# Attention inputs turned by VectorE instead of TensorE, head pair by head pair, in a fused attention and mixer kernel

## The chip, the cores and the metric

One core of one Trainium2 chip runs the whole program. The metric is the device time of one execution in microseconds. The kernel is timed as a median of several runs, and one execution is profiled.

## What is computed

Three layers, one after the other, for 4 batches of 768 positions. First a linear attention with a decay for every channel (8 heads of 48 channels), then an MLP mixer (over positions, then over channels), then a channel mix with a shift by one position.

```python
def _attn_ref(q, k, v, alpha):            # each (4, 8, 768, 48)
    for t in range(S):
        state = alpha[:, :, t, :, None] * state + np.einsum('bhd,bhe->bhde', k[:, :, t], v[:, :, t])
        y[:, :, t] = np.einsum('bhd,bhde->bhe', q[:, :, t], state)

def _moe_ref(x, w_tok1, w_tok2, w_ch1, w_ch2):    # x (4, 768, 384)
    u = x + (np.maximum(x.transpose(0, 2, 1) @ w_tok1, 0.0) @ w_tok2).transpose(0, 2, 1)
    return u + np.maximum(u @ w_ch1, 0.0) @ w_ch2

def _moe2_ref(x, mu_k, mu_r, w_k, w_v, w_r):
    xk = mu_k * x + (1.0 - mu_k) * x_prev         # x_prev is x one position earlier
    xr = mu_r * x + (1.0 - mu_r) * x_prev
    k = np.maximum(xk @ w_k, 0.0)
    return 1.0 / (1.0 + np.exp(-(xr @ w_r))) * (k * k @ w_v)
```

## The kernel before

Every engine has its own program, written out by hand. Nothing is scheduled; what stands in a program runs in that order, and semaphores tie the programs together.

**Steps.** The attention of one batch is cut into 24 steps: 6 chunks of 128 positions (`NC`) by 4 head pairs (`NP`). One step works on 128 positions of two heads, 96 channels (`W2`). `step(i)` gives chunk `i // 4` and head pair `i % 4`, so the four head pairs of a chunk follow each other and a state is needed again only four steps later. A step goes through these functions:

- TensorE `transposes` (L508): three matmuls with the identity turn q, k and alpha of the step, each from 128 positions x 96 channels to 96 x 128, into one bank. It raises `tr_done`.
- VectorE `scans` (L914, L916) makes running products of alpha forwards and backwards, `scale_qk` (L923, L926, L929) multiplies q and k by them into `qkd` and raises `qkd_ready`.
- ScalarE `spread_q` (L769 twice, L773) rounds q (for each head) and k to the high halves `qs_hi` and `ks_hi`; VectorE `split_low` (L939 twice, L943) makes the low halves `qs_lo` and `ks_lo`.
- TensorE `attention_scores`: a transpose of k (L522) and three matmuls (L530). It raises `scores_done`.
- VectorE `mask` (L949) copies the scores under the causal mask into `am`; ScalarE `store_kdt` (L763) copies the turned k.
- TensorE `attention_out`: scores times v (L546), q times state (L550, not in the first chunk) and k times v (L553, not in the last). It raises `y_done`.
- ScalarE `high_x` (L759) and VectorE `outputs` (L960 or L963 for the state, L968 for the low half of the result), then GpSimd `own_head` (L420) clears the other head's part of the state.

The first batch (`r = 0`) runs alone, with two banks for each kind of tile. Its part of the code stays as it is but for the signatures of the helper functions.

**Slots.** From batch `r = 1` on, the attention of batch r is interleaved with the mixer of batch r-1 in 28 slots. In a slot TensorE first does the mixer's part, then the attention's. Slot 0 has `token_up`, slots 1 to 3 have two tiles of `token_down` each (L602, L611), slots 4 to 27 have one tile of `channel_up` (L623, 9 matmuls) and, from slot 5, one of `channel_down` (L639, 9 matmuls). `steps_of` says which step each part of the attention is at: in slot s TensorE does `attention_out` of step s-2, `attention_scores` of step s-1 and `transposes` of step s. In slot 0 the attention's part comes ahead of the mixer's. VectorE does in a slot: the low half of the mixer's tile (`tile_low`, L993 or L995, which waits for ScalarE's high half, L777), `outputs` of step s-2, `scans` and `scale_qk` of step s, `mask` of step s-1, `split_low` of step s. Here the scores, the outputs and the turned inputs have one bank each. In slot 16 and behind slot 27 VectorE also reads three finished sums (`read_sums`, L1003).

**Loads.** SyncE's queue brings q, k, alpha and v by chunk: one DMA each of 128 partitions x 8 heads x 48 channels (L299, L306), rows of 192 bytes. The first batch uses three buffers, the later ones two. The first chunk of the second batch is loaded inside the loop over the first batch's slots, the second one right behind it (L344), the others in a loop on SyncE. The same queue brings pieces of the weights into `w_raw` (L315); each of these waits until GpSimd has split an earlier piece (L414, `w_lo_ready`).

After the three interleaved batches TensorE runs the mixer of the last batch alone and then the channel mix (L691, L700, L713), which the change doesn't touch.

## Time and profile before

| | |
|---|---|
| time, median of 3 runs | 775.81 us (774.6 to 778.8) |
| the profiled execution's own time | 774.48 us |
| its span in the profile | 772.6 us |
| TensorE busy | 758.6 us, 98% |
| VectorE busy | 467.7 us, 61% |
| ScalarE busy | 302.3 us, 39% |
| GpSimd busy | 127.5 us, 17% |
| granted TensorE clock | full (1.00) in every stretch read |

The span falls into stages. The first batch's attention runs until about 57 us. Then come three stretches of about 128.6 us, each with 28 slots, until about 443 us; behind them the last mixer until about 545 us and the channel mix until the end. An engine's busy share is a mean over all of these. The chain of work that ended last is followed back from the last instruction; an engine's share of it says for how much of the span this engine decided when things went on.

### The profile page before, as it was taken

How to read it: one execution, taken by the hardware profiler on the slowest of the kernel's cores; microseconds unless marked ns; L12 is line 12 of the kernel's file. 1: busy time of each engine (PE TensorE's matmuls, PEld its weight loads, DVE VectorE, ACT ScalarE, POOL GpSimd, SP SyncE). 2: the span in 40 equal slices, each digit the busy share in tenths (PEclk: the TensorE clock that was granted, in tenths of full speed). 3: DMA queues.
4: the chain of work that ended last, by engine and by line, in shares of the span. 5: the costliest groups of instructions: out<-in, count | busy, mean ns of one | idle time of the engine just before them, and what ended most of it. 6: DMA issues, size and time to landing. Idle time of an engine off the chain costs nothing.

```text
span 772.6 us, 13667 instructions
## 1 busy us (share of the span) xinstructions
PE 758.6 (98%) x4814; PEld 745.9 (97%) x4814; DVE 467.7 (61%) x1379; ACT 302.3 (39%) x843; POOL 127.5 (17%) x174
## 2 busy tenths in 40 slices
PE   7999999999999999999999999999899999999998
PEld 6888999999999999999999999999899999999998
DVE  7987777763877774577777331334573563663651
ACT  4664333331433332243333132235463553553641
POOL 2782532100123110012211052001000000000000
PEclk9999999999999999999999999999999999999999
DMA  9965222221222322022240015001010110110000
GB/s 208 215 166 99 42 43 42 73 42 41 42 43 42 72 42 42 31 42 42 42 128 1 1 59 173 32 1 62 19 44 31 41 51 31 41 51 31 10 21 31
DMA packets 114502, 43.77 MB, mean 57 GB/s; under 512 B 101776, under 2 KB 111632, under 8 KB 114448
## 3 DMA queue, kind: packets, MB, share of 16 engines
q1 hardware_dynamic: 111200, 37.96, 20.5%
q0 software_dynamic: 1152, 4.72, 1.7%
q10 hardware_dynamic: 2096, 0.39, 0.3%
q8 instruction: 31, 0.51, 0.3%
q14 instruction: 23, 0.19, 0.1%
HBM read 33.63 MB, written 9.44 MB: 56 GB/s over the span
## 4 chain that ended last, share of the span: by engine, by line
PE 85%; DVE 9%; ACT 3%; issue 1%; DMA 1%; SPq 1%; DVEq 0%; ACTq 0%
PE bank L639 19%; PE bank L623 19%; PE bank L713 13%; PE bank L691 12%; PE bank L700 4%; PE bank L546 3%; PE bank L530 3%; PE bank L508 3%; PE bank L550 2%; PE bank L580 2%; PE bank L611 1%; ACT qs_hi L769 1%; PE bank L553 1%; DVE qkd L929 1%; DVE qs_lo L939 1%
## 5 line engine op out<-in xcount | busy, mean ns | idle before, releaser
L769 ACT ACTIVATE qs_hi<-qkd,rhead 96x128 fp32r<-96x128 f32 x144 | 50.1, 395 | 152.1 <-DVE qkd L929 152.1
L993 DVE SCALAR_TENSOR_TENSOR hid_lo<-bank,hid_hi 128x384 fp32r<-128x384 f32 x96 | 52.8, 550 | 68.2 <-ACT hid_hi L777 68.2
L777 ACT ACTIVATE hid_hi<-bank 128x384 fp32r<-128x384 f32 x96 | 45.9, 479 | 68.9 <-PE bank L623 68.9
L420 POOL TENSOR_TENSOR state<-state,own 96x96 f32<-96x96 f32 x80 | 31.0, 387 | 248.4 <-DVE state L963 175.7
L623 PE MATMUL bank<-u_hi,wch_hi 128*128 128x384 f32 x288 | 71.4, 356 | 0.0
L869 ACT ACTIVATE relu_k<-bank 128x384 f32<-128x384 f32 x64 | 31.5, 492 | 101.2 <-PE bank L691 83.5
L939 DVE SCALAR_TENSOR_TENSOR qs_lo<-qkd,rhead,qs_hi 96x128 fp32r<-96x128 f32 x144 | 46.0, 359 | 35.6 <-ACT qs_hi L769 35.6
L623 PE MATMUL bank<-u_lo,wch_hi 128*128 128x384 f32 x288 | 65.8, 336 | 0.0
L639 PE MATMUL bank<-hid_lo,wch_hi 128*128 128x384 f32 x288 | 65.5, 335 | 0.0
L623 PE MATMUL bank<-u_hi,wch_lo 128*128 128x384 f32 x288 | 65.5, 335 | 0.0
L639 PE MATMUL bank<-hid_hi,wch_hi 128*128 128x384 f32 x288 | 65.5, 335 | 0.0
L639 PE MATMUL bank<-hid_hi,wch_lo 128*128 128x384 f32 x288 | 65.4, 334 | 0.0
L1109 DVE TENSOR_TENSOR x_half<-bank,x_half 128x384 f32<-128x384 f32 x24 | 13.4, 558 | 76.0 <-PE bank L713 74.7
L1092 DVE TENSOR_TENSOR relu_k<-relu_k 128x384 f32<-128x384 f32 x64 | 35.8, 559 | 27.8 <-ACT relu_k L869 25.0
L546 PEld LDWEIGHTS bank<-vt,relu_k 128*128 128x128 f32 x352 | 50.4, 190 | 1.8 <-DVE relu_k L949 1.8
L623 PEld LDWEIGHTS bank<-u_lo,wch_hi 128*128 128x128 f32 x288 | 51.6, 188 | 0.0
L623 PEld LDWEIGHTS bank<-u_hi,wch_lo 128*128 128x128 f32 x288 | 51.5, 188 | 0.0
L639 PEld LDWEIGHTS bank<-hid_hi,wch_hi 128*128 128x128 f32 x288 | 51.2, 188 | 0.1
L639 PEld LDWEIGHTS bank<-hid_hi,wch_lo 128*128 128x128 f32 x288 | 51.3, 188 | 0.0
L639 PEld LDWEIGHTS bank<-hid_lo,wch_hi 128*128 128x128 f32 x288 | 51.3, 188 | 0.0
L759 ACT ACTIVATE x_hi<-bank 128x96 fp32r<-128x96 f32 x96 | 23.8, 247 | 69.3 <-PE bank L553 52.9
L546 PE MATMUL bank<-vt,relu_k 128*128 128x48 f32 x352 | 47.9, 258 | 0.8 <-DVE relu_k L949 0.8
(118 smaller groups left out, 1777.1 us busy)
## 6 DMA issues: line engine op xcount, KB each, us to landing
w_raw<-in_moe_w_ch SPq DMA_DIRECT2D x12, 384.0 KB, 3.7
x_scratch<-x_half POOLq DMA_DIRECT2D x8, 576.0 KB, 3.5
out<-x_half SPq DMA_DIRECT2D x24, 192.0 KB, 1.9
qka<-in_q SPq DMA_DIRECT2D x21, 192.0 KB, 2.9
qka<-in_k SPq DMA_DIRECT2D x21, 192.0 KB, 3.5
qka<-in_alpha SPq DMA_DIRECT2D x21, 192.0 KB, 3.7
vt<-in_v SPq DMA_DIRECT2D x21, 192.0 KB, 2.7
qka<-x_scratch SPq DMA_DIRECT2D x4, 577.5 KB, 3.8
```

Of the source, the lines that this page charges most:

```text
L420: nc.gpsimd.tensor_tensor(state[0:W2, i % NP, :], state[0:W2, i % NP, :], own[0:W2, :], ALU.mult)\
L546: mm = nc.tensor.matmul(y_ps[:, h * D:(h + 1) * D], am[:, i % 2, h * P:(h + 1) * P], vt3[vb][:, p * W2 + h * D:p * W2 + (h + 1) * D], star ...
L623: mm = nc.tensor.matmul(dst, ch1_w(a, n % KC, jj), u[c][:, n % KC, half * HT:(half + 1) * HT], start=(n == 0), stop=(n == 3 * KC - 1))
L639: mm = nc.tensor.matmul(b_acc[m][:, 0:HT], ch2_w(a, jj, m), hid[c][:, j % HJ, :], start=(jj == 0 and n == 0), stop=(jj == NJ - 1 and n == 2))
L691: mm = nc.tensor.matmul(dst, wk_w(a, n % KC, j), mix_out[0][c][:, n % KC, :], start=(n == 0), stop=(n == 3 * KC - 1))
L713: mm = nc.tensor.matmul(bank[m][:, 0:DM], k2[a][:, n % NF, m * P:(m + 1) * P], wv_w(c, n % NF), start=(n == 0), stop=(n == 3 * NF - 1))
L769: nc.scalar.activation(dst[0:W2, h * P:(h + 1) * P], qkd[0:W2, first_of(i), :], ACT.Copy, scale=rhead[0:W2, i % 4, h:h + 1])\
L777: nc.scalar.activation(dst, b_ring[t % 2][:, 0:HT], func).then_inc(tile_hi, 1)
L869: nc.scalar.activation(relu_k[:, j % 2, :], b_ring[j % 2][:, 0:HT], ACT.Relu)\
L939: nc.vector.scalar_tensor_tensor(qs[1][0:W2, cols], qkd[0:W2, first_of(i), :], rhead[0:W2, i % 4, h:h + 1], qs[0][0:W2, cols], ALU.mult, A ...
L993: ins = nc.vector.scalar_tensor_tensor(dst, src, 0.0, hi, ALU.max, ALU.subtract)
L1092: nc.vector.tensor_tensor(relu_k[:, j % 2, :], relu_k[:, j % 2, :], relu_k[:, j % 2, :], ALU.mult).then_inc(k2_ready, 1)
```

## The change

From the second batch on:

- q, k and alpha are loaded by head pair and half of the positions (`load_half`, 384 positions) instead of by chunk. Such a half takes twelve DMAs for q, k and alpha, each of 32 partitions x 12 blocks, with rows of 32 or 16 channels (128 or 64 bytes), and two DMAs for v. They lay out the data so that every 32x32 block holds 32 positions on partitions and 32 channels in the row.
- VectorE turns all blocks of a step with one instruction, 96 partitions x 384 elements, into the bank into which TensorE's transposes went (`turn`, with the semaphore `turned`). TensorE's three transposes are gone.
- The order of the steps becomes head pair by head pair: `step` gives chunk `i % 6`, head pair `i // 6`. The state made by a step is needed by the next one. `add_x` can add up a chunk only in the last six steps.
- The parts of the attention are one slot earlier: in slot s `attention_out` of step s-1, `attention_scores` of step s, and the preparation (`turn`, `scans`, `scale_qk`, `spread_q`, `split_low`) of step s+1. Step 0 is prepared ahead of slot 0, behind the last slot of the batch before.
- The mask: ScalarE copies the scores into `am` (`store_scores`), GpSimd clears what lies in the future (`clear_future`). The low half of k moves from VectorE to GpSimd (`split_k`).
- All loads of the second batch stand behind the first batch's loop on SyncE's queue.

```diff
-            lags = (0, 2, 3) if is_first(r) else (0, 1, 2)
+            lags = (0, 2, 3) if is_first(r) else (-1, 0, 1)
...
+        GROUPS = ((0, 0, 0, 32, 0), (32, 0, 32, D, 0), (32, 1, 0, 64 - D, D - 32), (64, 1, 64 - D, D, 0))
...
+            def load_half(r, n):
...
+                if before < 2:
+                    sp.wait_ge(tr_done, NP * (4 + before))
+                else:
+                    sp.wait_ge(turned, TM * (before - 1))
+                ts = slice(half * HT, (half + 1) * HT)
+                for a, t in enumerate((q, k, alpha)):
+                    for lane, h, d0, d1, f0 in GROUPS:
+                        sp.dma_start(blocks[buf][lane:lane + 32, a, :, f0:f0 + d1 - d0],
+                                     t[r, 2 * p + h, ts, d0:d1].rearrange("(t p) d -> p t d", p=32))\
+                          .then_inc(qka_loaded[buf], 16)
...
-            load_qka(1, 1, 1)
-            load_v(1, 1, 1)
...
+            for r in range(1, B):
+                for n in range(HALVES):
+                    load_half(r, n)
...
+            def clear_future(r, i):
+
+                pool.wait_ge(am_copied, STEPS * (r - 1) + i + 1)
+                scores = am[:, i % 2, :].rearrange("p (h t) -> p h t", h=2)
+                nc.gpsimd.affine_select(out=scores, in_=scores, compare_op=ALU.is_ge, fill=0.0,
+                                        base=0, pattern=[[0, 2], [1, P]], channel_multiplier=-1).then_inc(am_ready, 1)
+
+            def split_k(r, i):
+                pool.wait_ge(ks_hi_ready, STEPS * (r - 1) + i + 1)
+                nc.gpsimd.tensor_tensor(ks[1][0:W2, :], qkd[0:W2, second_of(i), :], ks[0][0:W2, :], ALU.subtract)\
+                    .then_inc(ks_lo_ready, 1)
...
-                if tr is not None:
+                if is_first(r) and tr is not None:
                     transposes(r, tr)
...
+            def store_scores(r, i):
+
+                act.wait_ge(scores_done, STEPS * r + i + 1)
+                nc.scalar.activation(am[:, i % 2, :], scores_kdT(r, i)[0], ACT.Copy).then_inc(am_copied, 1)
...
+            def turn(r, i):
...
+                dve.wait_ge(qka_loaded[buf], loads)
+                dve.wait_ge(qkd_ready, STEPS * r + i)
+                nc.vector.transpose(transposed_qka(r, i),
+                                    blocks[buf][:, :, 4 * n:4 * (n + 1), :].rearrange("p a t f -> p a (t f)"))\
+                    .then_inc(turned, 1)
...
+            def prepare(r, i):
+                if not is_first(r):
+                    turn(r, i)
+                scans(r, i)
+                scale_qk(r, i)
+                if not is_first(r):
+                    split_low(r, i)
...
+            prepare(1, 0)
             for r in range(1, B):
                 for s in range(SLOTS):
                     mixer_part(r - 1, s)
                     attention_part(r, s)
                     if s == 0:
                         second_low(r - 1)
+                if r + 1 < B:
+                    prepare(r + 1, 0)
                 read_sums(r - 1, 1)
```

VectorE where the second batch begins (`omu` is the last thing of the first batch, `h_lo` and `u_lo` are low halves of the mixer's tiles, the `L914` of this stretch is the first scan). Before:

```order
L1061 TENSOR_SCALAR omu<-mu 128x6 [waits mu_loaded]
L993 SCALAR_TENSOR_TENSOR h_lo<-bank,h_hi 128x384 [waits tile_hi]
L914 SCALAR_TENSOR_TENSOR decays<-bank,mixed 96x128 [waits tr_done]
L916 SCALAR_TENSOR_TENSOR decays<-bank,mixed 96x127
L923 RECIPROCAL rlast<-decays 96x1 [waits decay_ready]
L926 TENSOR_SCALAR rhead<-bank,rlast 96x2 [waits rlast_ready]
L929 TENSOR_TENSOR qkd<-bank,decays 96x2x128 [waits suffix_ready]
```

and of the changed kernel:

```order
L1137 TENSOR_SCALAR omu<-mu 128x6 [waits mu_loaded]
L974 STREAM_TRANSPOSE bank<-qka 96x384 [waits qkd_ready,qka_loaded0]
L987 SCALAR_TENSOR_TENSOR decays<-bank,mixed 96x128 [waits turned]
L989 SCALAR_TENSOR_TENSOR decays<-bank,mixed 96x127
L996 RECIPROCAL rlast<-decays 96x1 [waits decay_ready]
L999 TENSOR_SCALAR rhead<-bank,rlast 96x2 [waits rlast_ready]
L1004 TENSOR_TENSOR qkd<-bank,decays 96x2x128 [waits scores_done,suffix_ready]
L1014 SCALAR_TENSOR_TENSOR qs_lo<-qkd,rhead,qs_hi 96x128 [waits qbd_ready,rhead_ready]
L1014 SCALAR_TENSOR_TENSOR qs_lo<-qkd,rhead,qs_hi 96x128
L1069 SCALAR_TENSOR_TENSOR h_lo<-bank,h_hi 128x384 [waits tile_hi]
```

The whole preparation of step 0 now stands ahead of the mixer's first low half.

SyncE's queue at the same place, from the last chunk's v of the first batch on. Before:

```order
L306 DMA mixed<-in_v 128x8x48 [waits y_done]
L315 DMA w_raw<-in_moe_w_ch 128x768 [waits w_lo_ready]
L299 DMA qka<-in_q 128x8x48 [waits tr_done]
L299 DMA qka<-in_k 128x8x48
L299 DMA qka<-in_alpha 128x8x48
L315 DMA w_raw<-in_moe_w_ch 128x2x384 [waits w_lo_ready] x2
L306 DMA vt<-in_v 128x8x48 [waits y_done]
L315 DMA w_raw<-in_moe_w_ch 128x2x384 [waits w_lo_ready] x4
L299 DMA qka<-in_q 128x8x48 [waits tr_done]
```

and of the changed kernel:

```order
L313 DMA mixed<-in_v 128x8x48 [waits y_done]
L345 DMA w_raw<-in_moe_w_ch 128x768 [waits w_lo_ready]
L345 DMA w_raw<-in_moe_w_ch 128x2x384 [waits w_lo_ready] x6
L328 DMA qka<-in_q 32x12x32 [waits tr_done]
L328 DMA qka<-in_q 32x12x16 x2
L328 DMA qka<-in_q 32x12x32
L328 DMA qka<-in_k 32x12x32
L328 DMA qka<-in_k 32x12x16 x2
```

The second batch's first q, k and alpha stood ahead of the last six pieces of `w_raw`, and stand behind them now.

One step of VectorE in the slots with `channel_up` and `channel_down`, in the changed kernel (`L1035` is the state, `L1040` the low half of the result):

```order
L1069 SCALAR_TENSOR_TENSOR hid_lo<-bank,hid_hi 128x384 [waits tile_hi]
L1035 SCALAR_TENSOR_TENSOR state<-state,decays,bank 96x96 [waits state_ready,xhi_ready]
L1040 TENSOR_TENSOR x_lo<-bank,x_hi 128x96
L974 STREAM_TRANSPOSE bank<-qka 96x384 [waits qkd_ready,qka_loaded1]
L987 SCALAR_TENSOR_TENSOR decays<-bank,mixed 96x128 [waits turned,state_sum]
L989 SCALAR_TENSOR_TENSOR decays<-bank,mixed 96x127
```

The transpose stands between the outputs of the step before and the scans; the mask and `ks_lo`, which stood behind L929, are gone from VectorE.

## Rows read from the trace of the kernel before

**Rows 1.** The page, chain that ended last: share of the span by engine.
```profile
PE 85%; DVE 9%; ACT 3%; issue 1%; DMA 1%; SPq 1%; DVEq 0%; ACTq 0%
```

**Rows 2.** The chain from 184 to 212 us: start us, us, engine and output.
```profile
187.71 0.32 DVE decays L914
...
194.09 0.33 DVE decays L914
...
198.28 0.33 DVE decays L914
...
202.46 0.33 DVE decays L914
...
206.11 0.33 PE bank L508 x3
206.44 1.56 PE bank L623 x9
...
209.56 0.38 PE bank L546 x4
...
210.24 0.38 PE bank L530 x3
```

**Rows 3.** Timeline in the second interleaved batch: start us, us, engine, line, op, [idle before].
```profile
261.98 0.33 PE L553 MATMUL bank<-vt,relu_k 128*96 128x96 f32 x2
...
263.27 0.30 DVE L963 SCALAR_TENSOR_TENSOR state<-state,decays,bank 96x96 f32<-96x96 f32 x1
...
267.97 0.42 DVE L914 TENSOR_TENSOR_SCAN decays<-bank,mixed 96x128 f32<-96x128 f32 x1
...
269.38 0.69 ACT L769 ACTIVATE qs_hi<-qkd,rhead 96x128 fp32r<-96x128 f32 x2 [2.02 <-DVE qkd L929]
...
269.98 0.30 ACT L773 ACTIVATE ks_hi<-qkd 96x128 fp32r<-96x128 f32 x1
270.17 0.61 DVE L939 SCALAR_TENSOR_TENSOR qs_lo<-qkd,rhead,qs_hi 96x128 fp32r<-96x128 f32 x2 [0.48 <-ACT qs_hi L769]
...
271.47 0.33 PE L553 MATMUL bank<-vt,relu_k 128*96 128x96 f32 x2
...
271.67 0.36 PE L530 MATMUL bank<-qs_hi,ks_hi 96*128 96x256 f32 x1
271.84 0.25 ACT L759 ACTIVATE x_hi<-bank 128x96 fp32r<-128x96 f32 x1 [1.06 <-PE bank L553]
...
272.12 0.31 DVE L963 SCALAR_TENSOR_TENSOR state<-state,decays,bank 96x96 f32<-96x96 f32 x1 [0.67 <-ACT x_hi L759]
272.35 0.24 DVE L968 TENSOR_TENSOR x_lo<-bank,x_hi 128x96 fp32r<-128x96 f32 x1
```

**Rows 4.** Groups by line over the whole span: count, busy us, mean ns of one.
```profile
L993 DVE SCALAR_TENSOR_TENSOR hid_lo<-bank,hid_hi 128x384 fp32r<-128x384 f32 x96 | 52.8, 550 | 68.2 <-ACT hid_hi L777 68.2
...
L420 POOL TENSOR_TENSOR state<-state,own 96x96 f32<-96x96 f32 x80 | 31.0, 387 | 248.4 <-DVE state L963 175.7 <-DVE state L960 72.7
...
L427 POOL TENSOR_TENSOR x_sum<-x_hi,x_lo 128x384 f32<-128x384 f32 x24 | 24.2, 1006 | 49.0 <-DVE x_lo L968 49.0
```

**Rows 5.** Timeline of SyncE's queue: start us, us, engine, line, transfer.
```profile
1.32 0.46 SPq L318 DMA_DIRECT2D qka<-in_alpha  x1
...
59.21 0.47 SPq L299 DMA_DIRECT2D qka<-in_q  x1
59.72 0.58 SPq L299 DMA_DIRECT2D qka<-in_k  x1
60.34 1.30 SPq L299 DMA_DIRECT2D qka<-in_alpha  x1
```

**Rows 6.** The page's DMA issues: count, KB each, us from issue to landing.
```profile
qka<-in_alpha SPq DMA_DIRECT2D x1, 48.0 KB, 2.6
```

**Rows 7.** Timeline of TensorE where slot 0 of the second batch begins.
```profile
56.57 0.49 PE L508 MATMUL bank<-ident,qka 128*96 128x128 f32 x3
```

**Rows 8.** The chain from 60 to 80 us, where slot 5 begins.
```profile
76.99 1.56 PE bank L623 x9
```

More of the change, by code:

```diff
@@ L446, in attention_part @@
             def attention_part(r, s):
-                i = steps_of(r, s)[2]
-                if i is not None and i < NST:
-                    own_head(r, i)
-                if i is not None and i % NP == NP - 1:
-                    add_x(r, i // NP)
+                tr, sc, yo = steps_of(r, s)
+                if yo is not None and step(r, yo)[0] < NC - 1:
+                    own_head(r, yo)
+                if not is_first(r):
+                    if sc is not None:
+                        clear_future(r, sc)
+                    if tr is not None:
+                        split_k(r, tr)
+                if yo is not None and step(r, yo)[1] == NP - 1:
+                    add_x(r, step(r, yo)[0])
             for s in range(SLOTS):
@@ L494, in transposes @@
             def transposes(r, i):
-                c, p = step(i)
-                qb, loads = chunk_buffer(r, c)
-                if is_first(r) and i == 0:
+                c, p = step(r, i)
+                qb, loads, _ = buffers(r, i)
+                if i == 0:
                     pe.wait_ge(consts_g, 3)
@@ L500, in transposes @@
                     pe.wait_ge(pair_loaded, 48)
-                if i % NP == (1 if is_first(r) and i < NP else 0):
-                    pe.wait_ge(qka_loaded[qb], 48 * loads)
-                if not is_first(r):
-                    pe.wait_ge(qkd_ready, STEPS * r + i)
-                elif i >= 2:
+                if i % NP == (1 if i < NP else 0):
+                    pe.wait_ge(qka_loaded[qb], loads)
+                if i >= 2:
                     pe.wait_ge(qkd_ready, i - 1)
@@ L531, in attention_scores, with v_of @@
                 mm.then_inc(scores_done, 1)
+            def v_of(r, i):
+                n = i % NP if is_first(r) else i % TM
+                return vt3[buffers(r, i)[0]][:, n * W2:(n + 1) * W2]
             def attention_out(r, i):
-                c, p = step(i)
+                c, p = step(r, i)
                 pe.wait_ge(am_ready, STEPS * r + i + 1)
-                vb, loads = chunk_buffer(r, c)
-                pe.wait_ge(v_loaded[vb], 16 * loads)
+                vb, _, loads = buffers(r, i)
+                pe.wait_ge(v_loaded[vb], loads)
                 y_ps, kv_ps = y_kv(r, i)
@@ L974, in attention_part @@
                         mask(r, sc)
[L975 to L980 removed]
+                    if tr is not None:
+                        prepare(r, tr)
                     if yo is not None:
@@ L983, in attention_part @@
                 else:
-                    if sc is not None:
-                        mask(r, sc)
+                    if yo is not None:
+                        outputs(r, yo)
                     if tr is not None:
-                        split_low(r, tr)
+                        prepare(r, tr)
             def tile_low(b, t, dst, hi, relu):
```

156 lines of the change are left out of this document (88 added, 68 removed).

## The prediction

> **What bounds the kernel now.** I read the chain of work that ended last first: 85% of the span is TensorE and 9% VectorE [rows 1]. The kernel ends when TensorE's list of work ends, plus the stretches in which TensorE waited. The chain itself shows both kinds of stretch. In the slots with the mixer's channel tiles it runs through TensorE alone: 3.12 us of mixer (206.44 to 209.56), 0.68 us of `attention_out` and the turned k, 0.38 us of scores, 0.33 us of transposes [rows 2]. With the state's matmuls on top (absent in that first chunk) such a slot is 4.74 us, from two slots that span 261.98 to 271.47 [rows 3]. In slots 1 to 3 the chain goes through VectorE and ScalarE: scans start at 194.09, 198.28 and 202.46, so 4.18 us for a slot in which TensorE has less to do [rows 2]. There a faster TensorE wins nothing and a longer VectorE loses.
>
> **What is removed.** The three transposes of a step take 0.33 us of TensorE's path [rows 2]. 24 steps x 3 batches x 0.33 = 23.8 us at most. That is the whole possible gain; the mask and the low half of k were not on TensorE's path. A channel slot would shrink from 4.74 to 4.41 us.
>
> **What is added to VectorE.** One transpose of 384 elements ahead of the scans, which wait for it. The trace has no such instruction. The nearest row is another 384-element operation, 0.55 us [rows 4]; I take 0.60 with the filling of a block, and 0.64 with the hand-over. From below 0.50 bounds it, from above 0.90 (the two qs_lo operations of 128 columns take 0.61, so 0.30 each, times three [rows 3]). The Trainium skill, VectorE: DVE Perf Modes, section on the three transpose paths, gives 311 ns for 128x128 bf16 on VectorE against 390 on TensorE, and its rule for authors sends a 128x128 turn to TensorE; an estimate from that page with 256 more columns at 0.96 GHz is 0.58 us. Against it the trace shows 0.11 us for each transpose inside TensorE's stream. By the page's prices VectorE's turn would look like a plain gain; by the rows it swaps 0.33 us of one engine for 0.6 us of another.
>
> **The loop in the channel slots.** This decides whether the 0.33 us come out. From the end of k times v (271.80) the changed order goes: `x_hi` ends 0.29 later, the state starts at 0.32 and `x_lo` at 0.55 [rows 3], the turn at 0.71, the scan at 1.35, ScalarE's spread 1.41 after it (267.97 to 269.38) at 2.76, its `ks_hi` ends 0.90 later (270.28) at 3.66. GpSimd then makes `ks_lo`: by its 0.387 for 96 elements and 1.006 for 384 [rows 4] 0.46 for 128, with 0.08 hand-over 4.20, and TensorE starts the scores at 4.27. In a slot of 4.41 us it could start them at 4.28 (today 0.13 before the modelled end of k times v, 271.67 against 271.80 [rows 3]). So the slack is 0.01 us: the channel slots just follow TensorE. Where the loop is longer by d, waits alternate and cost d/2 a slot. VectorE's own round has more room (0.67 us idle today [rows 3], plus 0.2 for `ks_lo`, minus 0.64, minus 0.33). GpSimd's 0.4 us for clearing the scores and its 1.0 us for a chunk's sum fall between two `split_k`; `own_head` is now needed a slot later and not four, and has over 2 us left. Two shortfalls remain. A last-chunk step has no k times v and no turned k: that slot is 0.3 us shorter and the loop is not, three per batch, 0.3 x 9 = +2.7 us. And in slot 16 the three reads of sums start the state 0.64 late (263.27 against 262.31 + 0.32 [rows 3]); today's slack swallows that, then nothing does: +1.9 us for three batches.
>
> **Slots 0 to 4.** They are on VectorE's round. A round loses `ks_lo` (0.20) and gains the turn (0.64): 4.63 instead of 4.19. In the third batch (`r = 2`) the chain has scan 0 at 187.71 [rows 2]. In the changed order scan 1 stands there, at 188.35. Scan 1 was at 194.09; now scan 2 comes there, later by 0.44 (h_lo behind the longer preparation), 0.33 (the outputs of step 0) and 0.64: 195.50. Two rounds more give scan 4 at 204.76; its `ks_lo` is ready 2.92 later, and with 0.38 of scores slot 5 begins at 208.06, not 206.44: +1.6 us. In return one step more is done by then. From slot 5 on TensorE saves 19 x 0.33 and that step's 0.59 + 0.47: 7.3 us. So a batch gains 5.7 us before the two shortfalls, for `r = 2` and 3.
>
> **The first interleaved batch** is different: its loads. They stood ahead of the last six weight pieces and were there in time; now they stand behind them on SyncE's queue, which gets past the last piece at 59.2 us (the next load of today starts at 59.21 [rows 5]). VectorE's turn of step 0 waits for all twelve DMAs, and behind it in VectorE's order stand the mixer's first low half and all else; TensorE stands before the scores of step 0, from 56.6 us on, where its transposes for that step begin today [rows 7]. An issue takes 0.50 us (0.46 and a gap, in the row of 256 rows a DMA; today's with 1024 rows 0.51 and 0.62) [rows 5], landing 2.6 us [rows 6]: 59.2 + 11 x 0.50 + 2.6 = 67.3 us. Bounds: 65.3 (0.37 a piece, 2.0) and 69.8 (0.62, 3.8). The turn ends at 68.0, so scan 0 starts at 68.05. From there: the low halves are ready 2.8 later (267.97 to 270.78 [rows 3]), the mixer's low half at 3.25, scan 1 at 3.9, scan 2 after 7.15 as in the other batches and 0.5 more since `token_up` of 3.1 us now starts only when the scores of step 0 are done, 11.55; two rounds and 3.3 more: slot 5 at 68.05 + 24.1 = 92.15 us instead of 76.99 [rows 8]: +15.2 us. TensorE is idle for some 14 us in one piece.
>
> **Steady loads.** A half is fourteen issues, about 7 us of queue and some 3 us to land, and there are four slots (17.6 us) between the last turn out of a buffer and the first out of its next filling. I take them as hidden. If an issue took over 1 us they would not be.
>
> **Sum.** +15.2 (first batch's start) + 3.2 (two other starts) - 22.0 (three times 7.3) + 2.7 + 1.9 = +1.0 us. On the execution's own 774.48 that is 775.5; the median of the runs is 1.3 above that execution, so 776.8.
>
> **Rivals.**
>
> A, the clock. For TensorE's 14 us of idleness there is no row: the trace has full clock throughout and no gap over 2 us in the interleaved part. If the granted clock falls to 1.2 GHz there, the scores and `token_up` (0.38 + 3.12) take up to twice as long; about 2 of these 3.5 us lie on the path to `h_lo`, since VectorE's preparation of step 1 covers the rest: 778.8. The Trainium skill, TensorE: Matmul & The Clock Gate, section on what is happening, says that the throttled state is the default and activity lifts it, which speaks for this rival. Chance 0.24, of which 0.10 end above 779.7.
>
> B, slower: the loop of the channel slots becomes VectorE's and GpSimd's. It decides as soon as the turn takes over 0.61 us, or `split_k` over 0.47. Near the upper bound, at 0.85 for the turn, d is 0.25: 0.12 x 51 slots = 6 us, and 0.25 x 9 rounds in slots 0 to 3 = 2 us: 785. At 0.72, 781. For it: the slack is 0.01 by rows. Against: 0.55 is the pace of every 384-element operation. Chance 0.22.
>
> C, faster: the loads land at 65.3 (-2.0), the turn takes 0.52 (-1 us over the rounds) and the loop's gain of 0.08 takes up most of the shortfalls (-3.5): 770.3. For it: small loads of today land in about 2 us when the queues are idle. Against: weight pieces are still in flight at 59 us. Chance 0.16.
>
> That the transposes go but the time stays is the forecast itself. Forecast: chance 0.38, of it 0.30 within the middle band, 0.03 below, 0.05 above.
>
> **Numbers.** A measurement can tell about 0.5%, 3.9 us, from no change. Faster 0.16 + 0.03 = 0.19; same 0.30 + 0.14 = 0.44; slower 0.22 + 0.10 + 0.05 = 0.37. Range: from C's 770.3 less 1.3 for an earlier start still to B's 785 and a little for A on top of B: 769 to 786.
>
> **What would show it.** No L508 group after 57 us and a VectorE transpose of 0.55 to 0.65 us, 72 times. The first of them between 65 and 70 us, with TensorE idle from 57 to about 71 and slot 5 at about 92. Channel slots of 4.4 us, with waits of TensorE on `ks_lo` of tenths at most, once per head pair. Starts of later batches in which VectorE's rounds are 4.6 us. Wrong would be: turns that wait for loads again and again, channel slots of 4.6 or more, or a first turn before 62 us.

## The result, and the profile after

The changed kernel takes 819.2 us (median of 4 runs, 818.5 to 819.8) against 775.8 us: ratio 1.055, 95% interval 1.052 to 1.058. That is 43.4 us slower. The prediction said 776.8 us, with 786 as the upper end of its range, so it was wrong. The profiled execution spans 818.1 us against 772.6. Its chain of the work that ended last, by engine and by line, answers to [rows 1]:

```profile
PE 61%; DVE 23%; issue 7%; ACT 6%; SPq 1%; DMA 1%; POOL 0%; DVEq 0%; ACTq 0%
PE bank L761 12%; PE bank L687 12%; PE bank L671 11%; PE bank L739 11%; DVE qs_lo L1014 4%; ACT qs_hi L826 4%; PE bank L748 4%; DVE bank L974 3%; DVE decays L987 3%; DVE qkd L1004 3%; DVE decays L989 2%; PE bank L628 2%; PE bank L573 2%; PE bank L659 2%; DVE hid_lo L1069 2%
```

TensorE had 85% of the chain and has 61%; VectorE went from 9% to 23%. The first group of the page is now VectorE's low half of q; before it was ScalarE's high half. Groups by line, with count, busy us and mean ns of one, and then idle time before and its releaser; the turn and the low half of k stand below it:

```profile
L1014 DVE SCALAR_TENSOR_TENSOR qs_lo<-qkd,rhead,qs_hi 96x128 fp32r<-96x128 f32 x144 | 88.6, 654 | 60.3 <-ACT qs_hi L826 60.3
...
L974 DVE STREAM_TRANSPOSE bank<-qka 96x384 f32<-96x384 f32 x72 | 41.5, 577 | 11.2 <-DMA qka<-in_alpha 11.0 <-issue 0.2
```

```profile
L457 POOL TENSOR_TENSOR ks_lo<-qkd,ks_hi 96x128 fp32r<-96x128 f32 x72 | 34.6, 481 | 176.5 <-ACT ks_hi L830 176.5
```

The same group before was this. Nothing in its code was changed:

```profile
L939 DVE SCALAR_TENSOR_TENSOR qs_lo<-qkd,rhead,qs_hi 96x128 fp32r<-96x128 f32 x144 | 46.0, 359 | 35.6 <-ACT qs_hi L769 35.6
```

**Where the time went, by batch.** `token_up` stands in the chain at the same place in every batch. The rows of before are the first token tile at the end of each interleaved batch (the fourth is the second tile of the last mixer):

```profile
181.32 3.12 PE bank L580 x18
309.95 3.12 PE bank L580 x18
438.60 3.12 PE bank L580 x18
443.28 3.12 PE bank L580 x18
```

and after, with one row ahead that has no counterpart above, the second tile in slot 0 of the first interleaved batch:

```profile
72.57 4.56 PE bank L628 x18
209.33 3.12 PE bank L628 x18
345.80 3.12 PE bank L628 x18
482.51 3.12 PE bank L628 x18
```

The first interleaved batch ends later by 209.33 - 181.32 = 28.0 us. The two others take 136.5 and 136.7 instead of 128.6 and 128.7, 15.9 together. The tail behind 482.51 is 1.6 longer. Sum 45.5 us, the difference of the spans. Of the first batch's 28.0 us 18.9 are there by slot 5 (95.84 against the 76.99 of [rows 8]), and the other 9.1 come from the slots behind it.

**Two slots of the same kind, side by side.** This is the reading that matters most. The timeline of the changed kernel holds a slot in which GpSimd has a 1.0 us sum queued behind the low half of k, and the next one, where it has not (start us, us, engine, line, operation, idle time before it):

```profile
284.61 1.76 DVE L1014 SCALAR_TENSOR_TENSOR qs_lo<-qkd,rhead,qs_hi 96x128 fp32r<-96x128 f32 x2 [0.83 <-ACT qs_hi L826]
...
284.80 0.48 POOL L457 TENSOR_TENSOR ks_lo<-qkd,ks_hi 96x128 fp32r<-96x128 f32 x1 [2.19 <-ACT ks_hi L830]
285.24 0.99 POOL L465 TENSOR_TENSOR x_half<-u_hi,u_lo 128x384 f32<-128x384 f32 x1
...
286.48 0.36 PE L573 MATMUL bank<-qs_hi,ks_hi 96*128 96x256 f32 x1 [0.72 <-issue]
...
290.04 0.81 DVE L1014 SCALAR_TENSOR_TENSOR qs_lo<-qkd,rhead,qs_hi 96x128 fp32r<-96x128 f32 x2 [0.83 <-ACT qs_hi L826]
...
290.22 0.48 POOL L457 TENSOR_TENSOR ks_lo<-qkd,ks_hi 96x128 fp32r<-96x128 f32 x1 [2.25 <-ACT ks_hi L830]
```

The pair of `qs_lo` took 0.61 us in [rows 3]. Here it takes 0.81 beside `ks_lo` alone: it ends at 290.85, 0.15 behind GpSimd. Beside `ks_lo` and the sum it takes 1.76 and ends at 286.37, again 0.14 behind GpSimd, which finishes at 286.23. The two are not stretched alike. The view of this line over the four `qs_lo` of both slots gives least, median and greatest ns of one:

```profile
L1014 DVE SCALAR_TENSOR_TENSOR qs_lo<-qkd,rhead,qs_hi x4: 347/442/1495, 284.6 to 290.3; 96x128 fp32r<-96x128 f32 x4
```

The first of a pair starts 0.18 us before `ks_lo`, takes its usual 347 ns and ends while `ks_lo` still runs; the whole stretch is in the second (537 and 1495 ns). Over the 72 pairs of the changed kernel 0.81 us is the length of 36, some 1.6 to 1.76 that of 33, and 3 are under 0.75. Before, 68 of the 72 were 0.61. The wait that the row of the scores shows as 0.72 of "issue" ends right after the pair does.

From one pair's start to the next it is 5.43 us (284.61 to 290.04), and 4.59 to the one after it, at 294.63. Less the pair, that is 3.67 and 3.78: VectorE's round is 3.7 us plus the pair of `qs_lo`. With 0.61 it would be 4.3, below the 4.41 that the prediction gave TensorE. With 0.81 it is 4.5, with 1.76 it is 5.4. In this batch the scores' starts are 4.25 to 4.62 us apart in most slots with a short pair (4.47 and 4.60 behind the pairs above), 5.20 to 5.57 in those with a long one. The long ones, a little under half of each batch, are those in which GpSimd adds up `u` or `x` or splits a late weight piece. The three of some 1.6 us are of the last kind, and what stands behind `ks_lo` there has one input only (L500, a copy of a weight piece). The pair ends 0.14 us behind that copy (100.38 against 100.24):

```profile
98.80 1.58 DVE L1014 SCALAR_TENSOR_TENSOR qs_lo<-qkd,rhead,qs_hi 96x128 fp32r<-96x128 f32 x2 [0.83 <-ACT qs_hi L826]
...
98.98 0.49 POOL L457 TENSOR_TENSOR ks_lo<-qkd,ks_hi 96x128 fp32r<-96x128 f32 x1 [2.24 <-ACT ks_hi L830]
99.42 0.82 POOL L500 CAST wch_hi<-w_raw 128x768 fp32r<-128x768 f32 x1
```

**Theory P.** An instruction of VectorE with two operands in SBUF cannot end while GpSimd runs a two-operand instruction on SBUF. (As worded it is too wide: it holds for a VectorE instruction that starts while GpSimd's is running, not for the first of a pair; and it asks too much of GpSimd's, since the copy above has one operand.) Its rival T: the turn on VectorE's round is what costs, and `qs_lo` is only longer because something else holds it. VectorE's operations with one operand in PSUM, the memory with the banks, speak for P. In the kernel before, the second scan below starts and ends within GpSimd's sum and takes the 0.39 us that it takes elsewhere:

```profile
268.15 1.00 POOL L427 TENSOR_TENSOR x_sum<-x_hi,x_lo 128x384 f32<-128x384 f32 x1
```

```profile
268.31 0.39 DVE L916 TENSOR_TENSOR_SCAN decays<-bank,mixed 96x127 f32<-96x127 f32 x1
```

`hid_lo` says little here: its mean is 548 ns, and 550 before [rows 4], but it stands behind the pair and so starts when GpSimd's sum is over (286.30 against 286.23). Only 5 of its 96 overlap a two-input instruction of GpSimd, and they take 543 to 558 ns.

Two further rivals were named before e1. S: the state, now needed by the next step, sets the slot. L: the loads with rows of 64 and 128 bytes do.

### The profile page after: what moved, and what is told of

Read it like the earlier page. It is cut to its first block, busy times and chain, and to the rows that moved or that the text cites. A ratio compares the mean times of both kernels' runs of the same rounds, so it can differ in the third digit from the quotient of the medians.

```text
span 818.1 us, 13704 instructions
## 1 busy us (share of the span) xinstructions
PE 755.0 (92%) x4598; PEld 735.7 (90%) x4598; DVE 504.3 (62%) x1307; ACT 329.2 (40%) x915; POOL 189.6 (23%) x318
## 4 chain that ended last, share of the span: by engine, by line
PE 61%; DVE 23%; issue 7%; ACT 6%; SPq 1%; DMA 1%; POOL 0%; DVEq 0%; ACTq 0%
PE bank L761 12%; PE bank L687 12%; PE bank L671 11%; PE bank L739 11%; DVE qs_lo L1014 4%; ACT qs_hi L826 4%; PE bank L748 4%; DVE bank L974 3%; DVE decays L987 3%; DVE qkd L1004 3%; DVE decays L989 2%; PE bank L628 2%; PE bank L573 2%; PE bank L659 2%; DVE hid_lo L1069 2%
## 5 line engine op out<-in xcount | busy, mean ns | idle before, releaser
L1014 DVE SCALAR_TENSOR_TENSOR qs_lo<-qkd,rhead,qs_hi 96x128 fp32r<-96x128 f32 x144 | 88.6, 654 | 60.3 <-ACT qs_hi L826 60.3
L457 POOL TENSOR_TENSOR ks_lo<-qkd,ks_hi 96x128 fp32r<-96x128 f32 x72 | 34.6, 481 | 176.5 <-ACT ks_hi L830 176.5
L929 ACT ACTIVATE relu_k<-bank 128x384 f32<-128x384 f32 x64 | 31.5, 491 | 102.7 <-PE bank L739 85.1
L671 PE MATMUL bank<-u_lo,wch_hi 128*128 128x384 f32 x288 | 67.4, 342 | 0.0
L671 PE MATMUL bank<-u_hi,wch_hi 128*128 128x384 f32 x288 | 66.8, 340 | 0.0
L573 PE MATMUL bank<-qs_hi,ks_hi 96*128 96x256 f32 x72 | 25.9, 359 | 39.7 <-DVE qs_lo L1014 21.0
L573 PEld LDWEIGHTS bank<-qs_hi,ks_hi 96*128 96x128 f32 x72 | 13.5, 188 | 48.1 <-issue 41.1
L816 ACT ACTIVATE relu_k<-bank 128x256 f32<-128x256 f32 x72 | 27.7, 384 | 61.9 <-PE bank L573 61.8
```

The costliest lines, as they stand in the source:

```text
L457: nc.gpsimd.tensor_tensor(ks[1][0:W2, :], qkd[0:W2, second_of(i), :], ks[0][0:W2, :], ALU.subtract)\
L573: mm = nc.tensor.matmul(scores, ks[a][0:W2, :], qs[b][0:W2, :], start=(n == 0), stop=(n == 2))
L671: mm = nc.tensor.matmul(dst, ch1_w(a, n % KC, jj), u[c][:, n % KC, half * HT:(half + 1) * HT], start=(n == 0), stop=(n == 3 * KC - 1))
L1014: nc.vector.scalar_tensor_tensor(qs[1][0:W2, cols], qkd[0:W2, first_of(i), :], rhead[0:W2, i % 4, h:h + 1], qs[0][0:W2, cols], ALU.mult, A ...
```

## Experiments on the contention

**e1: the low half of k back on VectorE,** all else as changed.

```diff
-                    if tr is not None:
-                        split_k(r, tr)
...
                                                    ALU.mult, ALU.subtract).then_inc(split_ready, 1)
+                dve.wait_ge(ks_hi_ready, STEPS * (r - 1) + i + 1)
+                nc.vector.tensor_tensor(ks[1][0:W2, :], qkd[0:W2, second_of(i), :], ks[0][0:W2, :], ALU.subtract)\
+                    .then_inc(ks_lo_ready, 1)
...
```

> The changed kernel with one part undone: VectorE makes the low half of k again, GpSimd no longer does. Theory P (port): VectorE's qs_lo, which reads two SBUF operands, waits for the end of GpSimd's ks_lo and of the 1.0 us sum queued right behind it. Then qs_lo falls from a mean of 654 ns to 350, channel slots from 5.4 us to 4.4 to 4.6, the second and third interleaved batch from 136.6 to about 126 us, the time to 780 to 788 us. Rival S (the state made serial by the new order of steps sets the slot) and rival L (loads of 64 and 128 byte rows): slots stay near 5.4 us and the time stays above 810 us, while only the mean of qs_lo changes.

Measured 791.9 us (791.8 to 792.1), ratio 1.019 (1.016 to 1.022): 27.3 us back, though VectorE has an instruction more in every step. Its group of `qs_lo`:

```profile
L1009 DVE SCALAR_TENSOR_TENSOR qs_lo<-qkd,rhead,qs_hi 96x128 fp32r<-96x128 f32 x144 | 45.5, 355 | 60.5 <-ACT qs_hi L821 60.5
```

355 ns, as before the change. The slots are 4.25 to 4.6 us apart. The time is above the 780 to 788 us that P expected, so something else is left. The serial state and the loads are as in the changed kernel, so S and L are out as the cause of the slots over 5 us.

**e2: GpSimd's long instructions first.** `add_x`, `split_late` and `prepare_x2` are issued ahead of `clear_future` and `split_k`; the low half of k stays on GpSimd.

```diff
+                if r == 1 and FIRST_UNIT <= s < FIRST_UNIT + NMIX - NEARLY:
+                    split_late(NEARLY + s - FIRST_UNIT)
+                if BASE_SLOT <= s < BASE_SLOT + 2 * KC:
+                    prepare_x2(r - 1, s - BASE_SLOT)
                 if sc is not None:
                     clear_future(r, sc)
                 if tr is not None:
                     split_k(r, tr)
```

> The changed kernel with GpSimd's order in a slot changed: the long two-operand instructions (the chunk's sum, the base of the output, the late weight pieces) stand ahead of the clearing of the scores and of ks_lo instead of behind ks_lo. Theory P: qs_lo then only waits for the 0.48 us of ks_lo, its pair is 0.81 us in every slot (mean about 450 ns), slots of over 5 us vanish, the time is 783 to 795 us. If it is GpSimd's ks_lo by its result arriving late, or rivals S or L: no change from 819.

Measured 795.2 us (793.6 to 796.9), ratio 1.023 (1.019 to 1.027). Of the pairs 64 are now 0.81 us, 2 are 0.76 and 3 are 1.76. No work was taken away anywhere: the order alone brought back 24 us. It also shows what the move of `ks_lo` is worth at best. VectorE loses 0.20 for `ks_lo` and pays 0.20 for the stretched pair, and e1 and e2 are 3 us apart.

**e5: the kernel before, with only the low half of k moved to GpSimd.**

```diff
+                if not is_first(r) and steps_of(r, s)[0] is not None:
+                    split_k(r, steps_of(r, s)[0])
...
-                nc.vector.tensor_tensor(ks[1][0:W2, :], qkd[0:W2, second_of(i), :], ks[0][0:W2, :], ALU.subtract)\
-                    .then_inc(split_ready, 1)
...
```

> The kernel before with one thing moved: the low half of k is computed by GpSimd instead of VectorE (after GpSimd's state product of the slot), nothing else of the change. Theory P (VectorE's two-operand qs_lo cannot end while GpSimd runs a two-operand instruction on SBUF): the qs_lo pair goes from 0.61 to at least 0.81 us, the mean of one qs_lo from 359 ns to 440 or more, and because VectorE's round has only 0.01 us of slack against the slot the kernel gets slower: 0.28 us leave VectorE's round and 0.20 to 0.55 come back, and where GpSimd's 1.0 us sum follows, 1.15: a total of 778 to 795 us. Theory T (the turn on VectorE, not GpSimd's part in it, stretches the round): qs_lo stays at 359 ns, the round gets shorter, 770 to 777 us.

Measured 795.0 us (793.4 to 796.8), ratio 1.023 (1.020 to 1.026), 18 us slower than the kernel before. This kernel has no turn, so T is out as the cause of the longer pairs: the mean of `qs_lo` is 677 ns. Its timeline:

```profile
247.92 1.77 DVE L948 SCALAR_TENSOR_TENSOR qs_lo<-qkd,rhead,qs_hi 96x128 fp32r<-96x128 f32 x2 [0.48 <-ACT qs_hi L778]
248.10 0.49 POOL L449 TENSOR_TENSOR ks_lo<-qkd,ks_hi 96x128 fp32r<-96x128 f32 x1 [2.35 <-ACT ks_hi L782]
248.56 0.98 POOL L435 TENSOR_TENSOR x_half<-u_hi,u_lo 128x384 f32<-128x384 f32 x1
...
253.02 1.77 DVE L948 SCALAR_TENSOR_TENSOR qs_lo<-qkd,rhead,qs_hi 96x128 fp32r<-96x128 f32 x2 [0.48 <-ACT qs_hi L778]
```

The pairs are 5.10 us apart where they are long. Behind the pairs of 0.81 at 269.28 and 274.04 the scores are 4.74 and 4.76 apart, TensorE's own pace as in [rows 3]. So in this order of work a slot hides the 0.2, but not the 1.15, though `ks_lo` is gone from VectorE.

The trace of the kernel before already held the effect, in one of its four longer pairs, and I had not read it:

```profile
58.72 1.84 POOL L414 TENSOR_TENSOR wch_lo<-w_raw,wch_hi 128x768 fp32r<-128x768 f32 x1
...
60.15 0.82 DVE L939 SCALAR_TENSOR_TENSOR qs_lo<-qkd,rhead,qs_hi 96x128 fp32r<-96x128 f32 x2 [0.84 <-ACT qs_hi L769]
```

P stands, with the two corrections made above: the VectorE instruction that is stretched is the one that starts second, and GpSimd's need only read SBUF. The Trainium skill, SBUF — State Buffer, section "SBUF: two separate sides", says that VectorE and GpSimd share a pair of ports as "an exclusive lock, not a bandwidth split": a VectorE operation with two SBUF inputs or a GpSimd operation that reads SBUF, whichever starts first, has it for the whole instruction, and the other is fully blocked. The rows agree as far as VectorE goes: the pair takes 0.81 and 1.76 us where it was 0.61, its first `qs_lo` keeps its 347 ns, and the scan, which reads a bank, is not stretched. That GpSimd waits for VectorE's first `qs_lo` in full they do not show: `ks_lo` takes 0.44 to 0.46 us where it runs beside no `qs_lo` that started earlier, and 0.48 to 0.50 beside one that runs on for 0.17 us of it.

## Experiments on the late loads and the clock

**e3: the first half's q, k and alpha early,** on SyncE's queue in slot 16 of the first batch's loop, ahead of the last weight pieces.

```diff
+                if s == NP * (NC - 2):
+                    load_half(1, 0, "q")
+                if s == NP * (NC - 2) + 3:
+                    load_half(1, 0, "v")
...
-                for n in range(HALVES):
+                for n in range(1 if r == 1 else 0, HALVES):
```

> The changed kernel with the first half's q, k and alpha of the second batch issued inside the first batch's loop again, ahead of the last weight pieces, and v three slots later. Theory: the 11 us in which VectorE's first turn waits for its DMAs vanish, and with them TensorE's idle stretch and the drop of its granted clock to half: the first turn at about 58 us instead of 67.9, time 800 to 804 us (15 to 18 less). If the first batch's start cost nothing on the path, the time stays at 819.

Measured 810.4 us (809.6 to 811.2), ratio 1.043 (1.039 to 1.046): 8.8 us back, about half of the 15 to 18 that I expected. **e4** makes both edits, e1's and e3's.

> Both edits: low half of k on VectorE and early loads of the first half. Theory P with the start: the two gains add, 762 to 771 us, faster than the kernel before (775.8). If the serial state or the loads limit the slots, it stays above 785 us.

Measured 783.85 us (782.1 to 784.4), ratio 1.008 (1.005 to 1.011). The two edits add up (27.3 and 8.8 make 36.1, measured 35.3), but the kernel is still slower than before, against every expectation of mine. Its timeline at the second batch's start shows where a part of what the loads gave was lost again:

```profile
56.79 0.58 DVE L975 STREAM_TRANSPOSE bank<-qka 96x384 f32<-96x384 f32 x1
...
57.86 3.57 POOL L438 TENSOR_TENSOR wch_lo<-w_raw,wch_hi 128x768 fp32r<-128x768 f32 x2
...
59.60 2.23 DVE L1015 SCALAR_TENSOR_TENSOR qs_lo<-qkd,rhead,qs_hi 96x128 fp32r<-96x128 f32 x2 [0.83 <-ACT qs_hi L827]
...
62.19 0.55 PE L574 MATMUL bank<-qs_hi,ks_hi 96*128 96x256 f32 x1 [2.93 <-DVE ks_lo L1019]
```

The turn is 11 us earlier than the 67.86 of the changed kernel. But its pair of `qs_lo` now meets GpSimd's last two weight pieces and takes 2.23 us, TensorE waits 2.93 us, and its matmuls run at the lower clock besides. Windows of TensorE (from and to, length, busy us and count, granted clock, DMA share, GB/s), of the changed kernel:

```profile
54.00:76.00 22.00, 8.96 (x36) 0.53 0.58 107
76.00:96.00 20.00, 17.28 (x118) 1.00 0.23 31
96.00:99.00 3.00, 3.00 (x12) 0.51 0.28 33
```

The clock's second fall, at 96 us, costs there too: the first tile of slot 5 takes 2.60 us in the chain and not 1.56. In e4 the granted clock is 0.70 over 54 to 76 us.

**e7: e4 with TensorE kept busy there,** by idle matmuls: 3 more in each of the last four slots of the first batch's loop and 24 after it.

```diff
+                if s >= SLOTS - 4:
+                    keep_warm(3)
...
             early_token_up(NC - 1)
+            keep_warm(24)
```

> The fourth variant (783.85 us) with 3 idle matmuls of 128 columns more in each of the last four slots of the first batch's loop and 24 after it, which keep TensorE busy while it waits for the second batch's first pair; the computation is the same. Rival A (the clock is what the first batch's end and the second's start lose): the granted clock stays at 1.00 through 54 to 68 us, token_up takes 3.1 instead of 5.05 us, the scores 0.59 instead of 0.78: 3 to 4 us less, 780 to 781 us. If the clock falls all the same, or the time is lost in waits, 783 to 786.

Measured 782.7 us (781.4 to 783.6), ratio 1.007 (1.005 to 1.010), 1.2 less than e4, which is not clear of noise (the runs of e4 lie between 782.1 and 784.4). The window shows that the clock was held at 2.4 GHz there (it fell later, from 86 to 89 us), and the chain that `token_up` takes 3.15 us instead of e4's 5.05:

```profile
54.00:76.00 22.00, 21.57 (x164) 1.00 0.43 89
```

```profile
64.56 3.15 PE bank L629 x18
```

It starts 1.39 later than in e4 (63.17), since the idle matmuls were too many and ran until 64.09. From the scores' start to the end of `token_up` it is 6.03 us in e4 and 3.54 in e7. So up to 2.5 us of this batch's start are the clock's, and 0.5 were won there. Rival A of the prediction came true as a mechanism, and it is a small term.

## Experiments on the turn

What is left in e4 is the turn itself. Its slots are 4.52 us apart where TensorE would need less, with VectorE idle only while ScalarE makes `qs_hi`, 0.83 us. One turn is 0.58.

**e6: the next pair's turn in that gap.** e4, with `turn(r, i + 1)` issued between `scale_qk` and `split_low` of step i instead of ahead of the scans of step i+1.

```diff
-                if not is_first(r):
+                if not is_first(r) and i == 0:
                     turn(r, i)
                 scans(r, i)
                 scale_qk(r, i)
                 if not is_first(r):
+                    if i + 1 < STEPS:
+                        turn(r, i + 1)
                     split_low(r, i)
```

> The fourth variant (low half of k on VectorE, first loads early; 783.85 us) with the turn of the next pair issued right behind q*k*decay of this pair, so that it runs in the 0.83 us in which VectorE waits for ScalarE's qs_hi; one turn is 0.58. If what is left over the kernel before is the turn on VectorE's round, the channel slots fall from 4.52 to TensorE's own 4.24 us, slots 2 to 4 and the read_sums slot by 0.6 each: 17 x 0.28 + 4 x 0.6 = 7.2 us a batch in three batches, 783.9 - 21.5 = 762 us (758 to 768), faster than the kernel before. If what is left are the stretches at the lower clock and the starts of the batches, the slots stay at 4.5 and the time at 779 to 785.

Measured 762.3 us (762.25 to 762.6), ratio 0.981 (0.980 to 0.983). That is 21.5 us less than e4, as worked out, and 14 us faster than the kernel before. The state is as serial in e6 as in the changed kernel, and its loads have the same short rows: S and L do not set its slots either. The timeline:

```profile
252.66 0.69 ACT L827 ACTIVATE qs_hi<-qkd,rhead 96x128 fp32r<-96x128 f32 x2 [1.08 <-DVE qkd L1005]
252.73 0.59 DVE L975 STREAM_TRANSPOSE bank<-qka 96x384 f32<-96x384 f32 x1
253.46 0.61 DVE L1015 SCALAR_TENSOR_TENSOR qs_lo<-qkd,rhead,qs_hi 96x128 fp32r<-96x128 f32 x2
...
254.85 0.36 PE L574 MATMUL bank<-qs_hi,ks_hi 96*128 96x256 f32 x1
255.30 0.31 DVE L1039 SCALAR_TENSOR_TENSOR state<-state,decays,bank 96x96 f32<-96x96 f32 x1 [0.56 <-ACT x_hi L808]
```

The turn runs beside `qs_hi`, `qs_lo` starts at its old distance behind it, and VectorE now has 0.56 us of idleness in front of the state: TensorE is the bound again. From slot 4 to the last one of this batch 19 slots take 82.9 us, 4.36 each.

**e11, e12, e13** fill the table: the same move of the turn in the changed kernel itself, in e1 and in e3. Their edits are those shown.

> The changed kernel (819.2 us) with one thing moved: the turn of the next pair is issued behind q*k*decay of this one, into VectorE's 0.83 us gap; the low half of k stays on GpSimd and the loads stay late. Theory P with the round as the bound: VectorE's round is shorter by 0.6 us in about 60 slots, down to TensorE's 4.25 at the least; slots that were 5.2 to 5.6 become 4.6 to 5.0, those at 4.4 to 4.6 become 4.25: 819 - 60 x 0.55 = 786 us (776 to 792). If the stretched qs_lo were the only thing that counts and the turn were covered, 815 to 819.

> The changed kernel with two things moved: the low half of k back to VectorE and the next turn in VectorE's gap; the first loads stay late (they stood at 60.0 us). 762.3 us of the variant that has the early loads as well, plus the 8.1 us that these were worth between the first and the fourth variant: 770.4 us (769 to 772), still faster than the kernel before (776.7).

> The variant that reached 762.3 us with the low half of k again on GpSimd (so: the changed kernel with early first loads and the next turn in the gap). Theory P: qs_lo is stretched as in the changed kernel (mean about 650 ns), but VectorE's round is now 4.52 - 0.58 - 0.28 = 3.66 us plus the stretch: 3.9 in plain slots, under TensorE's 4.25, so nothing shows there; 4.8 in the 9 or so slots of a batch in which GpSimd's 1.0 us sums or the weight pieces follow: 9 x 0.5 x 3 = 13 us, 770 to 776. If the contention were gone with the turn out of the way, 760 to 763.

Medians in us:

| | turn ahead of the scans | turn in the gap | difference |
|---|---|---|---|
| ks_lo on GpSimd, loads late | 819.2 (changed kernel) | 782.7 (e11) | -36.5 |
| ks_lo on GpSimd, loads early | 810.4 (e3) | 773.6 (e13) | -36.8 |
| ks_lo on VectorE, loads late | 791.9 (e1) | 772.2 (e12) | -19.7 |
| ks_lo on VectorE, loads early | 783.85 (e4) | 762.3 (e6) | -21.5 |

e11 has a ratio of 1.009 (1.006 to 1.011), e12 0.994 (0.993 to 0.996), e13 0.995 (0.993 to 0.997). The loads are worth 8 to 10 us in every row pair. The turn and the contention are not independent: having `ks_lo` on GpSimd costs 27 us with the turn on the round (changed kernel less e1, e3 less e4) and 10.5 to 11.3 with it in the gap (e11 less e12, e13 less e6). The reason is the round. In e13 the mean of `qs_lo` is still 669 ns:

```profile
L1020 DVE SCALAR_TENSOR_TENSOR qs_lo<-qkd,rhead,qs_hi 96x128 fp32r<-96x128 f32 x144 | 90.6, 669 | 12.2 <-ACT qs_hi L832 3.0
```

But a round of 3.7 - 0.58 + 0.81 = 3.9 us hides below TensorE's 4.36. With the long pair it is 4.9, and the slots there are 4.5 to 5.0 apart. In the second interleaved batch, with 10 long pairs, it is 106.85 us from the first scores to the last, against 103.14 in e6: 3.7 us, and three times that is 11.1.

## Experiments on the order in slot 0

**e9: TensorE's second token tile ahead of the scores of the first pair,** on e4; **e10** the same on e6.

```diff
-                attention_part(r, 0)
-                mixer_part(r - 1, 0)
-                for s in range(1, SLOTS):
+                for s in range(SLOTS):
                     mixer_part(r - 1, s)
                     attention_part(r, s)
```

> The fourth variant (783.85 us) with TensorE's order in slot 0 of each batch changed: the mixer's second token tile ahead of the scores of the first pair instead of behind them. At the start of the second batch TensorE then has 3 to 5 us of matmuls in the 2.93 us in which it waits for ks_lo (58.8 to 62.2 us): -3 to -4 us there; in the other two starts the h_hi and h_lo waits of slot 1 (0.49 + 0.19) go: -0.7 each. Total 778 to 780 us. If the scores were the later of the two anyway, 783 to 785.

> The variant that reached 762.3 us (low half of k on VectorE, first loads early, next turn in VectorE's gap) and TensorE's second token tile ahead of the first pair's scores in slot 0 of a batch. On the variant without the gap that order was worth 2.0 us, at the start of the second batch. If the two are independent: 760.3 us (759 to 761.5). If the turn in the gap already makes the scores the earlier of the two, 762 to 763.

e9: 781.8 us (780.7 to 783.3), ratio 1.007 (1.004 to 1.009), 2.0 less than e4 where I expected 4 to 6; the runs of the two overlap (e4: 782.1 to 784.4). e10: 763.1 us (762.4 to 764.1), ratio 0.983 (0.980 to 0.986), not faster than e6. The order gives at most little, and nothing once the turn is in the gap. No run shows why; e6 is the fastest version.

## Why the prediction was wrong, by its own steps

- **Transposes out of TensorE's path, 0.33 a step:** right. In e6, where TensorE sets most slots, the batches take 121.5 us (182.38 to 303.86) instead of 128.6. That is 7.1, where the step promised 0.33 x 24 = 7.9 at most.
- **One turn, 0.60 us, bounds 0.50 and 0.90:** right, 577 ns x72. The estimate of 0.58 from the Trainium skill, VectorE: DVE Perf Modes, section on the three transpose paths, agrees with it too. The page's comparison of engines does not decide here, as the prediction said. What decided was where on VectorE's round the 0.58 stood.
- **`ks_lo` on GpSimd, 0.46:** right as a duration, 481 ns. The failed step is what it does to others. The paragraph on the loop took ScalarE's and GpSimd's times and left `qs_lo` at the 0.61 of [rows 3], as if GpSimd's instruction beside it cost nothing. It asked whether GpSimd's 1.0 us sums delay `ks_lo`, that is, it looked at GpSimd's own queue. They stand behind `ks_lo`, so they do not; but they stand beside `qs_lo`. The term was 0, and it is at least 27.3 us (changed kernel against e1, which pays `ks_lo` on VectorE besides).
- **The loop's slack of 0.01 us:** no run shows the loop without contention, but VectorE's round without it would be 4.3 us against 4.41, so little slack was right. But I took it as the reason for rival B to need a longer turn or a longer `split_k`. A slack of 0.01 is gone by any stretch of anything on the loop, and rival B should have been priced by the chance of any such stretch. B's place was right, its mechanism and its price (8 us) were not.
- **"VectorE's own round has more room":** wrong, and by its own numbers: 0.67 + 0.2 - 0.64 - 0.33 is -0.10, no room at all. It was wrong as a way of counting too. The 0.67 us before the state [rows 3] is room. The 0.83 in front of `qs_lo` is not: it is the answer time of ScalarE, and the round has to go through it unless other work is put there. In e1 VectorE's round, with `ks_lo` back on it, is 4.52 us with only that idleness.
- **Slots 0 to 4 on a longer round:** predicted 4.63, measured 4.64, 4.87 and 4.93 between the scores of slots 1 to 4, a mean of 4.81, of which 0.2 is the stretched pair. Right but for the pair.
- **The first interleaved batch:** predicted first turn at 67.4, measured 67.86; issues 0.50 apart (2.00 and a gap for four, from 60.02), landing 2.2 us on the page instead of 2.6. Slot 5 was predicted at 92.15 and came at 95.84. Of the 3.7 us 0.4 are the loads (scan 0 at 68.48, predicted 68.05), 1.44 `token_up` at the lower clock (4.56 against 3.12) and 0.39 the scores (0.98 against 0.59). The other 1.4 no run takes apart; the stretched pairs are among them, 0.2 each. As a price of late loads, +15.2 was too high: the early loads win 8 to 10 us. In e4 a part of what they gain is lost again in the pair of 2.23 us and TensorE's wait of 2.93.
- **Steady loads hidden:** right. The turn's group shows 11.0 us of waiting for a DMA, and 11.04 are the very first one's:

```profile
67.86 0.59 DVE L974 STREAM_TRANSPOSE bank<-qka 96x384 f32<-96x384 f32 x1 [11.04 <-DMA qka<-in_alpha]
```

- **Shortfalls of the last-chunk steps and of slot 16:** the scores around the reads of the sums are 6.01 us apart, 1.4 more than the pair ahead of them, where 0.64 was allowed. VectorE's round was the bound, so nearly all of the three reads (1.47 us in e4) showed. The term for the last-chunk steps, +2.7, no run takes apart.
- **Rival A, the clock:** came true, 0.53 mean granted clock over 54 to 76 us. The price of about 2 us was fair: from the scores' start to the end of `token_up` it is 5.54 us (71.59 to 77.13), and 3.54 in e7 at the full clock. Not foreseen were the short later falls. The granted clock was 0.5 in part of 96 to 99 us and 0.66 on the mean over 163 to 168, and the first two mixer tiles of that slot took 4.71 us and not 3.12.

Together: with the contention taken out and `ks_lo` back on VectorE (e1) the kernel is 15 to 16 us over the one before. 8 us of that are the loads (e1 less e4), and the turn on a round that was already full costs 20 (e1 less e12); against them stands what the missing transposes give. The turn and the contention fill the same round. The forecast of +1.0 was missed by 42 us. The larger part is the contention, which was set at nothing; the rest is spread over the starts, the reads of the sums and the later falls of the clock. No run has the changed kernel with only the contention taken out, so how near the other terms would have come together stays open, and no run puts the mask back on VectorE.

## What to carry to other kernels

Before an instruction is moved to GpSimd, list what VectorE runs in the same microsecond: in these runs an operation of VectorE with both inputs in SBUF that starts while GpSimd reads SBUF was stretched until GpSimd's run of back-to-back instructions paused, and what stands behind the moved instruction counts as much as the instruction. When two engines hand work to and fro, an engine's idle time inside the round is either slack or answer time; answer time can be filled with work for the next step (0.58 us of turn in a gap of 0.83 was worth 21.5 us), and only slack can be spent. Where a computed slack is a hundredth of a microsecond, its loss is the likeliest case and not a rival.

## What the runs showed of the hardware that I had not expected

- A `qs_lo` takes 335 to 351 ns undisturbed. One that starts while GpSimd reads SBUF ends 0.14 to 0.15 us behind the last of GpSimd's back-to-back instructions, if that is later than its usual end. GpSimd's next instruction, if it follows at once, mostly goes ahead of the waiting `qs_lo`; in the two pairs of 0.76 us of e2 `qs_lo` got in between the clearing of the scores and the `ks_lo` behind it. Where the second of a pair is hit, the pair takes 0.81 or 1.76 us instead of 0.61. Where the first is hit, beside two weight pieces of 1.8 us, the pair takes 2.23, and the second one follows at its usual length. One input of GpSimd's instruction is enough, as the copy shows. The scans, with an operand in a bank, were not stretched: in the kernel before, 42 of 96 second scans ran for 0.3 of their time or more beside a two-input instruction of GpSimd and took 384 to 393 ns. Nor was the turn, which has one input in SBUF (72 turns of 573 to 591 ns, of which 58 beside such an instruction):

```profile
287.14 0.39 POOL L439 TENSOR_TENSOR state<-state,own 96x96 f32<-96x96 f32 x1 [0.92 <-DVE state L1035]
287.16 0.57 DVE L974 STREAM_TRANSPOSE bank<-qka 96x384 f32<-96x384 f32 x1
```

- The granted clock fell to 0.50 around the start of the second batch in every variant but e7: between 53 and 56 us in most, e5 included, whose list of work for TensorE up to there is the kernel before's, and only at 60 to 61 us in e11, e12 and e13. In the profiled execution of before it stayed at 1.00, with TensorE busy 0.43 of the microsecond from 52 to 53 us. In e5 it was busy 0.32 of the one from 53 to 54, and the next two rows of its windows are at 0.86 and 0.50:

```profile
54.00:55.00 1.00, 1.00 (x9) 0.86 0.00 0
55.00:56.00 1.00, 1.00 (x6) 0.50 0.63 75
```

Of the 27 executions of the kernel before that were timed together with the variants, 24 have a mean granted clock below 1.000, 23 of them 0.993 to 0.998. They too had stretches at the lower clock, which the one trace read for the prediction has not. So the first fall is not made by the change alone, and what decides it stays open. That it lasted until 76 us went with TensorE's idleness (8.96 us busy of 22).
